# Attention scores from re-paired operand copies, double buffered, with the copies made by VectorE for ten heads and by DMA for 22

## The reference

```
scores = q @ k.T / 8 + min(cum[j] - cum[i], 0), cum = cumsum(max(s, 0)); -1e9 above the diagonal
attn   = softmax(scores);  out = attn @ v
```

## Time and profile before

| what | value |
|---|---|
| median of 3 runs | 968.08 us (964.08 to 968.49) |
| the profiled execution | 964.65 us, its span 962.9 us |
| TensorE busy | 911.1 us, 95% of the span |
| VectorE, ScalarE busy | 487.5 us (51%), 351.8 us (37%) |
| DMA | 159.34 MB, 165 GB/s |
| mean granted TensorE clock | 0.985 of 2.4 GHz |

### The profile page before, as it was taken

How to read it: one execution, slowest core, us unless ns; L and a number is a source line. 1 busy time by engine, 2 the same in 40 slices (tenths; PEclk the granted TensorE clock), 3 DMA queues, 4 the chain that set the end, 5 groups by cost and what they waited for, 6 DMA issues and landing times.

```text
span 962.9 us, 16180 instructions
## 1 busy us (share of the span) xinstructions
PE 911.1 (95%) x6455; PEld 856.4 (89%) x6455; DVE 487.5 (51%) x889; ACT 351.8 (37%) x670; POOL 37.7 (4%) x80
## 2 busy tenths in 40 slices
PE   1999899998999999999999999999999999999998
PEld 1777688977999999988999999989899999999998
DVE  5546779345554882445433784055534690342222
ACT  1445566344333642444232443243422341221111
POOL 2011000000000000001000000000000000000000
PEclk9979999997999999999999999999999999999999
DMA  4667565752664563745545445544655444444441
GB/s 96 155 186 228 158 162 179 235 181 66 218 226 160 175 207 116 250 131 159 191 150 176 150 131 169 175 131 119 206 187 176 173 150 159 175 149 164 176 175 50
DMA packets 70562, 159.34 MB, mean 165 GB/s; under 512 B 31892, under 2 KB 46228, under 8 KB 58200
## 3 DMA queue, kind: packets, MB, share of 16 engines
q1 hardware_dynamic: 68184, 154.66, 51.0%
q0 software_dynamic: 2304, 3.65, 1.3%
HBM read 118.11 MB, written 30.09 MB: 154 GB/s over the span
## 4 chain that ended last, share of the span: by engine, by line
PE 80%; DVE 10%; issue 3%; ACT 3%; SPq 1%; DMA 1%; ACTq 0%; DVEq 0%
PE psum L1101 21%; PE psum L1103 20%; PE psum L1102 20%; PE psum L1078 8%; PE psum L1024 3%; PE psum L1057 2%; PE psum L1055 2%; DVE neg_max L799 2%; PE psum L1038 1%; DVE work L865 1%; PE psum L1029 1%; PE psum L1062 1%; DVE sums L825 1%; DMA klc<-cum_scratch 1%; DVE work L868 1%
## 5 line engine op out<-in xcount | busy, mean ns | idle before, releaser
L1101 PE MATMUL psum<-uu_hl,ring 128*128 128x288 f32 x512 | 156.7, 306 | 6.3 <-DVE r_hl L908 2.1
L1101 PE MATMUL psum<-r_hl,ring 128*128 128x288 f32 x512 | 155.2, 303 | 2.1 <-ACT hid L666 1.1
L1103 PE MATMUL psum<-uu_hl,ring 128*128 128x288 f32 x512 | 152.0, 297 | 0.0
L1102 PE MATMUL psum<-uu_hl,ring 128*128 128x288 f32 x512 | 151.8, 296 | 0.0
L1103 PE MATMUL psum<-r_hl,ring 128*128 128x288 f32 x512 | 151.2, 295 | 0.0
L1102 PE MATMUL psum<-r_hl,ring 128*128 128x288 f32 x512 | 151.1, 295 | 0.0
L799 DVE TENSOR_REDUCE neg_max<-psum 128x1 f32<-128x512 f32 (+4 forms) x165 | 83.5, 539 | 106.7 <-PE psum L1029 100.7
L1078 PE MATMUL psum<-probs,va 128*128 128x320 f32 (+4 forms) x448 | 125.1, 390 | 2.7 <-ACT probs L629 2.7
L908 DVE SCALAR_TENSOR_TENSOR r_hl<-psum,r_hl 128x288 fp32r<-128x288 f32 x128 | 58.5, 457 | 125.0 <-ACT r_hl L712 124.5
L712 ACT ACTIVATE r_hl<-psum 128x288 fp32r<-128x288 f32 x128 | 52.5, 411 | 183.3 <-PE psum L1103 183.2
L1101 PEld LDWEIGHTS psum<-uu_hl,ring 128*128 128x128 f32 x512 | 97.4, 190 | 9.8 <-DVE uu_hl L903 3.7
(11 more groups left out here) (102 smaller groups left out, 1684.6 us busy)
## 6 DMA issues: line engine op xcount, KB each, us to landing
ring<-w_scratch SPq DMA_DIRECT2D x72, 1024.0 KB, 4.9
w_scratch<-ring SPq DMA_DIRECT2D x24, 1024.0 KB, 5.5
kq_raw<-in_kq_t SPq DMA_DIRECT2D x70, 288.0 KB, 4.2
stage<-in_w_ch SPq DMA_DIRECT2D x16, 512.0 KB, 4.9
khc<-khh SPq DMA_DIRECT2D x34, 144.0 KB, 2.3
qm<-qhl SPq DMA_DIRECT2D x34, 144.0 KB, 2.5
out_t<-u_acc SPq DMA_DIRECT2D x16, 288.0 KB, 5.8
va<-in_v SPq DMA_DIRECT2D x34, 128.0 KB, 3.8
```

Of the source, the lines that this page charges most:

```text
L1101: pe.matmul(o, hi, m_hi, start=start, stop=False)
L1102: pe.matmul(o, hi, m_lo, start=False, stop=False)
L1103: return pe.matmul(o, lo, m_hi, start=False, stop=stop)
```

## The change

- `khc`, `klc`, `khh`, `qhl`, `qm` become `kb`, `qb` (128 partitions) and `kc`, `qc` (97 partitions), all double. Now `kb` is k's low part above its high part, `qb` q's high part above its low part; `kc` and `qc` hold the high parts, two rows of cum, and in partition 96 the row of the maximum, rows between being constant. The scores are kb x qb + kc x qc; `max_scores` uses 66 rows of `kc` and `qc`, so cum has to be loaded into one place only. `kq_raw` is double.
- The high parts reach `kc` and `qc` by two VectorE copies (`highs`) for heads 0 to 9, in step 3, and for heads 10 to 31 by two DMAs (`load_highs`) issued in step 4 behind `load_v`; `max_scores` waits for them in the next step 0.
- The low parts are computed in step 3 (before: 2); `load` is issued in step 0 (before: 3), cum in step 2 alone.
- The maxima are not split: they are rounded to fp32r as they are written, and each transpose has a stationary operand of one column and gives one row.
- TensorE's order: scores 0, round 0, scores 1, round 1 in g = 0; values 0, scores 2, round 2 in g = 1; the transposes in g = 3, ahead of values 2. `keep_warm` is gone.
- The small loads (taps, U, V) move from before head 1 to step 4 of head 0, their splitting from (0, 3) to (2, 4). At the start both heads' k and q are loaded first.
- Nothing is done for heads past the last.

```diff
-        KROWS = D + 4
-        kq_raw = sb("kq_raw", [P, 2, S], F32)
-        k_raw, q_raw = kq_raw[:, 0, :], kq_raw[:, 1, :]
-        khh = [sb(f"khh{i}", [P, S], F32R) for i in range(2)]
-        qhl = [sb(f"qhl{i}", [P, S], F32R) for i in range(2)]
-        klc = [sb(f"klc{i}", [KROWS, S], F32R) for i in range(2)]
-        qm = [sb(f"qm{i}", [KROWS, S], F32R) for i in range(2)]
-        khc = sb("khc", [KROWS, S], F32R)
+        CROWS, KROWS = D + 2, 3 * P // 4 + 1
+        kq_raw = sb("kq_raw", [P, 2, 2, S], F32)
+        kb = [sb(f"kb{i}", [P, S], F32R) for i in range(2)]
+        qb = [sb(f"qb{i}", [P, S], F32R) for i in range(2)]
+        kc = [sb(f"kc{i}", [KROWS, S], F32R) for i in range(2)]
+        qc = [sb(f"qc{i}", [KROWS, S], F32R) for i in range(2)]
         va = [sb(f"va{i}", [P, NT, P], F32) for i in range(2)]
         probs = sb("probs", [P, 2, BANK], F32)
-        neg_max = sb("neg_max", [P, 8], F32)
-        max_split = sb("max_split", [P, NT, P], F32R)
+        neg_max = sb("neg_max", [P, 8], F32R)
+        WEIGHTS_HEADS = [1, 2, 4, 6]
+        SMALL_AT = (0, 4)
+        COPIED = H + 2
+        UV_AT = (2, 4)
                 def load(a, h):
-                    n = a * H + h
-                    ql_done.wait(sp, n - 1)
-                    kl_done.wait(sp, n - 1)
+                    n, i = a * H + h, h % 2
+                    if n >= B * H:
+                        return
+                    if n >= 2:
+                        ql_done.wait(sp, n - 2)
+                        kl_done.wait(sp, n - 2)
                     for half in (0, D):
-                        sp.dma_start(kq_raw[half:half + D, :, :], kq_t[source(a, h)]).then_inc(raw_in.sem, 16)
+                        sp.dma_start(kq_raw[half:half + D, i, :, :], kq_t[source(a, h)]).then_inc(raw_in[i].sem, 16)
                 def load_v(a, h):
                     n, i, c0 = a * H + h, h % 2, D * (h % 2)
+                    if n >= B * H:
+                        return
                     mm_pv.wait(sp, n - 2)
                     of = v[source(a, h)]
                     sp.dma_start(va[i][:, 0:NT - 1, c0:c0 + D],
                                  of[0:(NT - 1) * P, :].rearrange("(t p) d -> p t d", p=P)).then_inc(v_in[i].sem, 16)
                     sp.dma_start(va[i][P - D:P, NT - 1, c0:c0 + D], of[(NT - 1) * P:S, :]).then_inc(v_in[i].sem, 16)
-                def side(a, h):
+                def load_cum(a, h):
+                    n = a * H + h
+                    if n >= B * H:
+                        return
+                    mm_s.wait(sp, n - 2)
+                    sa, sh = source(a, h)
+                    sp.dma_start(kc[h % 2][D:D + 2, :].bitcast(F32), cum_scratch[sa * H + sh]).then_inc(cum_in.sem, 16)
+                def load_highs(a, h):
                     n, i = a * H + h, h % 2
+                    if n >= B * H:
+                        return
                     prep_hi.wait(sp, n)
-                    mm_max.wait(sp, n - 1)
-                    mm_s.wait(sp, n - 2)
-                    sp.dma_start(khc[0:D, :].bitcast(F32), khh[i][0:D, :].bitcast(F32)).then_inc(side_in.sem, 16)
-                    sp.dma_start(qm[i][0:D, :].bitcast(F32), qhl[i][0:D, :].bitcast(F32)).then_inc(side_in.sem, 16)
-                    sa, sh = source(a, h)
-                    cum = cum_scratch[sa * H + sh]
-                    sp.dma_start(khc[D + 2:D + 4, :].bitcast(F32), cum).then_inc(side_in.sem, 16)
-                    sp.dma_start(klc[i][D + 2:D + 4, :].bitcast(F32), cum).then_inc(side_in.sem, 16)
+                    sp.dma_start(kc[i][0:D, :].bitcast(F32), kb[i][D:2 * D, :].bitcast(F32)).then_inc(high_in.sem, 16)
+                    sp.dma_start(qc[i][0:D, :].bitcast(F32), qb[i][0:D, :].bitcast(F32)).then_inc(high_in.sem, 16)
+                def load_small():
...
                 def attention_step(a, h, g):
+                    if g == 0:
+                        load(a, h + 3)
                     if g == 2:
-                        side(a, h + 2)
-                    if g == 3:
-                        load(a, h + 3)
+                        load_cum(a, h + 2)
                     if g == 4:
                         load_v(a, h + 2)
+                        if a * H + h + 2 >= COPIED:
+                            load_highs(a, h + 2)
...
+                load(0, 0)
+                load(0, 1)
                 load_v(0, 0)
-                prep_hi.wait(sp, 0)
-                sp.dma_start(khc[0:D, :].bitcast(F32), khh[0][0:D, :].bitcast(F32)).then_inc(first_side, 16)
-                sp.dma_start(qm[0][0:D, :].bitcast(F32), qhl[0][0:D, :].bitcast(F32)).then_inc(first_side, 16)
-                load(0, 1)
-                for x, done in enumerate((s_cumh, s_cuml)):
-                    sp.wait_ge(done, 1)
-                    if x == 0:
-                        sp.wait_ge(s_rows, 3)
-                    row = y_hl[0][0:1, x, :].bitcast(F32)
-                    sp.dma_start(khc[D + 2 + x:D + 3 + x, :].bitcast(F32), row).then_inc(first_side, 16)
-                    sp.dma_start(klc[0][D + 2 + x:D + 3 + x, :].bitcast(F32), row).then_inc(first_side, 16)
+                for h in range(2):
+                    sp.wait_ge(s_rows1 if h else s_rows, 3)
+                    for x, done in enumerate((s_cumh, s_cuml)):
+                        sp.wait_ge(done, 1)
+                        sp.dma_start(kc[h][D + x:D + x + 1, :].bitcast(F32), y_hl[0][h:h + 1, x, :].bitcast(F32))\
+                          .then_inc(first_cum[h], 16)
...
+                    if (h, g) == SMALL_AT:
+                        load_small()
...
-                    raw_in.wait(act, n)
+                    if n >= B * H:
+                        return
+                    raw_in[i].wait(act, n // 2)
                     mm_s.wait(act, n - 2)
-                    act.activation(khh[i][:, :], k_raw, ACT.Copy).then_inc(prep_hi.sem, 1)
-                    act.activation(qhl[i][:, :], q_raw, ACT.Copy, scale=SCALE).then_inc(prep_hi.sem, 1)
+                    act.activation(kb[i][:, :], kq_raw[:, i, 0, :], ACT.Copy).then_inc(prep_hi.sem, 1)
+                    act.activation(qb[i][:, :], kq_raw[:, i, 1, :], ACT.Copy, scale=SCALE).then_inc(prep_hi.sem, 1)
                 def max_to_row(a, h):
                     n = a * H + h
+                    if n >= B * H:
+                        return
                     mm_mt.wait(act, n)
-                    act.activation(qm[h % 2][D:D + 2, :], psf[D:D + 2, MX:MX + S], ACT.Copy).then_inc(mrow.sem, 1)
+                    act.activation(qc[h % 2][KROWS - 1:KROWS, :], psf[0:1, MX:MX + S], ACT.Copy).then_inc(mrow.sem, 1)
...
+                    if g == 3:
+                        max_to_row(a, h + 1)
+                        prepare(a, h + 2)
                     if g == 4:
-                        max_to_row(a, h + 1)
...
-                def query_low(a, h):
+                def highs(a, h):
                     n, i = a * H + h, h % 2
+                    prep_hi.wait(dve, n, 1)
+                    dve.tensor_copy(kc[i][0:D, :], kb[i][0:D, :].bitcast(F32)).then_inc(copied.sem, 1)
                     prep_hi.wait(dve, n)
-                    dve.scalar_tensor_tensor(out=qhl[i][D:2 * D, :], in0=q_raw[D:2 * D], scalar=SCALE,
-                                             in1=qhl[i][D:2 * D, :].bitcast(F32), op0=ALU.mult, op1=ALU.subtract)\
+                    dve.tensor_copy(qc[i][0:D, :], qb[i][0:D, :].bitcast(F32)).then_inc(copied.sem, 1)
+                def lows(a, h):
+                    n, i = a * H + h, h % 2
+                    if n >= B * H:
+                        return
+                    if n < COPIED:
+                        copied.wait(dve, n, 1)
+                    else:
+                        prep_hi.wait(dve, n)
+                    dve.tensor_tensor(kb[i][0:D, :], kq_raw[0:D, i, 0, :], kb[i][0:D, :].bitcast(F32), ALU.subtract)\
+                       .then_inc(kl_done.sem, 1)
+                    dve.scalar_tensor_tensor(out=qb[i][D:2 * D, :], in0=kq_raw[D:2 * D, i, 1, :], scalar=SCALE,
+                                             in1=qb[i][D:2 * D, :].bitcast(F32), op0=ALU.mult, op1=ALU.subtract)\
                        .then_inc(ql_done.sem, 1)
-                def key_low(a, h):
-                    n = a * H + h
-                    mm_s.wait(dve, n - 2)
-                    dve.tensor_tensor(klc[h % 2][0:D, :], k_raw[0:D], khh[h % 2][0:D, :].bitcast(F32), ALU.subtract)\
-                       .then_inc(kl_done.sem, 1)
                 def maxima(a, h, r):
...
-                    if r == len(ROUNDS) - 1:
-                        red.wait(dve, n)
-                        dve.tensor_copy(max_split[:, :, D], neg_max[:, 0:NT]).then_inc(ms_hi.sem, 1)
-                        ms_hi.wait(dve, n)
-                        dve.tensor_tensor(max_split[:, :, D + 1], neg_max[:, 0:NT], max_split[:, :, D].bitcast(F32),
-                                          ALU.subtract).then_inc(ms_lo.sem, 1)
```

(62 more changed lines are left out.)

90 lines of the change are left out of this document (46 added, 44 removed).

## The result

The changed kernel takes 998.41 us (median of 4 runs, 996.64 to 999.54) against 966.92 us for the kernel before (4 runs, 964.08 to 968.49, on the same chip): a ratio of 1.034, 95% interval 1.032 to 1.037. It is slower, by more than the 990 forecast and within the range. The profiled execution took 997.98 us, span 995.8.

What follows compares the result with a forecast made beforehand. TensorE was taken as the bound from batch 1 on, a ring through three engines in batch 0. 964.65 - 5.2 + 2.6 - 8.1 + 27 + 8.4 = 989.4, given as 990 us; range 952 to 1011, forecast's own 975 to 1003.

Steps and rivals of the forecast that it cites:

- Start, -5.2: Up to the first scores: cum row issued and landing 4.7 us earlier, two splits gone; range -6 to -3.
- Batch 0, +2.6: Batch 0: 85.6 us against 83.0, paced by a ring through three engines; range -12 to +8.
- 2.0 over all: Batch 0: cum rows issued late, behind the 12 small loads or a stored block, cost 2.0 us in total.
- One stretch of 10.2: Batch 0: one stretch of 10.2 us at 0.50 clock, costing 5.1 us as before.
- ring: Batch 0: chain of dependent steps through three engines, 8.3 us per head, 66.4 us for eight heads.
- a head below 8: Batch 0: sign against the forecast, which is wrong if a head takes less than 8 us.
- Saved in batches 1 to 3, -8.1: Batches 1 to 3: round 2 and maximum-row waits go, transposes get shorter, maxima past the last head go; -8.1 us.
- The 2.9 for the maxima: Batches 1 to 3: three waits for line 799 go because round 2 moves a step later; 2.9 us saved.
- High parts by DMA, +27: Heads 10 to 31: step-4 DMAs behind `load_v` make TensorE wait; 31.1 us less 4 taken back, bounds 12 and 36.
- 14 for blocks: Seven of 22 DMA heads have a 0.5 to 1 MB load or store just ahead: 2 us each, 14.
- Clock, +8.4: Batches 1 to 3: three stretches of 10.2 us at half clock (15.3) instead of one costing 6.9; bounds -7 and +30.
- the clock goes with each wait: Rival, batches 1 to 3: new waits bring 1.2 GHz after nearly each, +30 us, 1011 us in all; chance 0.12.

Runs made afterwards that it cites:

- the fastest kernel: The changed kernel with batch 0's SyncE list rearranged, high-part DMAs in step 3, and heads 23 and 31 copied by VectorE: 954.16 us, ratio 0.9885.
- the other order of the list: The changed kernel with batch 0's small loads and weight blocks issued in step 2 behind the cum rows, instead of step 4: 983.24 us, ratio 1.017.
- the early DMAs: The changed kernel with the high-part DMAs issued in step 3 instead of step 4 behind the loads of v: 969.26 us, ratio 1.003.
- The two experiments: Keep-warm products put into the changed kernel with rearranged list and step-3 DMAs: 957.88 us, ratio 0.992; taken out of the kernel before: 975.12 us, ratio 1.009.

## Why the prediction was right, and where it was off

It was right in direction and in its largest term, and the total is 8 us short.

- **Start, -5.2.** Measured -6.3, just outside the range of -6 to -3. First product at 9.80, 6.2 before that of the earlier trace rows, so earlier than the near 11 I gave.
- **Batch 0, +2.6: the mis-sized step.** Measured +9.2, outside its range of -12 to +8. "2.0 over all" for late cum rows was 10.9, two waits of 5.4 and 5.6. I had seen both their causes (behind the small loads, behind a stored block) and priced the row at a quick landing. "One stretch of 10.2", 5.1, is in fact four (three are shown above), some 34 us at half clock, 27.0 of them busy; by half of the busy time (see the clock, below) some 13 is lost, an estimate. Set against the fastest kernel, which has 6.8 us at half clock in this batch and is busy 65.1, TensorE's 74.3 are 9.2 more. With the other order of the list cum cost 1.4 and the clock came to 0.89: both go together. The rest of my sum was too large and hid part of the miss: ring and additions without cum and low clock were 78.5, but the fastest kernel ran the whole batch in 75.1, with 1.3 of cum and some low clock in it. The second head, free of all additions on VectorE, took 8.1 beside the ring's 8.3, and the fifth, with two of a normalisation's, 7.8. I had said that a head below 8 would make the forecast wrong: one was, by 0.2, and it made no difference, so that test was drawn too tight.
- **Saved in batches 1 to 3, -8.1.** The rest of the kernel after the last head's start is 1.6 shorter (1.8 had been taken for the head past the last). Five transposes are 0.2 shorter (0.54 against 0.75 in the heads shown) where I took 0.1; over 23 heads that makes near 5 in place of 2.3. The 2.9 for the maxima had a wrong reason: round 2 stands one step behind round 1 in both kernels, so the order doesn't take that wait away. In the changed kernel it is near nothing (0.2), while round 0 waits for its DMAs; with the early DMAs 3.1 of it are back. Idle time of TensorE rose by 22.4 though the new waits are 29.8, so 7.4 of other waits went in all, where I had taken off 2.9, 1.1 and 4.
- **High parts by DMA, +27.** The waits are 29.8; my gross sum was 31.1, of which 4 were to be taken back. They stand at the heads named, and 1.0 each at two more. The experiment with the early DMAs confirms the chain that the term was built of: the two loads of v, the issues, the landing (2.68 to the use in the head shown, 2.5 in the earlier trace rows). The split was less good than the sum: the ten heads waited 27.7 where I had 17.1, and the other twelve 2.1. Values 3 to round 0 took 54.1 over the ten, where 41 stood in the sum, so most of what I had put down as 14 for blocks seems to have fallen on the ten. At heads 2 and 4 of batch 1 a block's store is issued just before `load_v` (166.44, 224.03), and values 3 to round 0 took 7.6 and 9.0 instead of the 4.3 of the head shown. The 2.3 us that the prediction adds from the Trainium skill (DMA: Bandwidth & Descriptors, on the anatomy of one DMA) are from a fit that the section gives for DMAs issued by GpSimd. These are issued by SyncE, and their medians are 2.5 before and 3.0 after, so the measurement decides.
- **Clock, +8.4: close by luck.** TensorE's busy time in heads 8 to 31 rose by 9.3, with ten stretches (58 us in all) at half clock instead of two (17). I had three stretches of 10.2, 30.6, and took half of their length. Most are short, 3.4 or 6.8, and nine of the ten begin beside a new wait or within 2 us behind it (one of the nine, at 224, was there before too). So of the rival "the clock goes with each wait" the mechanism largely came, but not its price of 30. What a stretch costs can be read off products of one shape in one of them and just behind it (the clock goes from 0.50 to 1.00 at 152.4; start, duration):

```profile
151.27 0.44 PE L1122 MATMUL psum<-x_hl,ring 128*128 128x288 f32 x1
151.51 0.44 PE L1123 MATMUL psum<-x_hl,ring 128*128 128x288 f32 x1
...
152.57 0.29 PE L1122 MATMUL psum<-x_hl,ring 128*128 128x288 f32 x1
152.71 0.29 PE L1123 MATMUL psum<-x_hl,ring 128*128 128x288 f32 x1
```

From start to start it is 0.24 at half clock and 0.14 at full. So near half of the busy time in a stretch is lost, and none of its idle time. TensorE is busy 47.2 of the 58 us (before: 15.6 of 17), 31.6 more; half is some 14 to 16, an estimate. The shorter transposes hide near 5 of that in the 9.3. My 8.4 for the clock and my 2.3 for the transposes were both too small, by amounts that partly cancel.
- **Heads 8 to 31 in sum.** The last three terms make 27.3; the ghost head's -1.8 lies behind the last head, so 29.1 stands against the 31.6 measured.
- **Keep-warm.** I took their 10.7 us of busy time as free gain beside the ring. The two experiments agree with this for the new order alone; in the old one they are worth 0.9%.

What stays open: how the 4.5 us which heads 8 to 31 still lack with the early DMAs divide (2.6 are idle time, 1.9 busy time, with 38 us at half clock instead of 17); what brings the clock down, in a list without long waits above all; and how much of batch 0's spread from 75.1 to 79.5 is chance, since each profile is one execution.

## What to carry to other kernels

A transfer has to be issued its whole latency ahead of its use, counted from where it stands in its queue's list and not from when its data is ready; here moving two issues one step, with the same bytes, was worth 27 us of 31.6. A few rows that the main engine needs go ahead of the bulk in the list, for a 4.5 KB row behind two megabytes took 8 us and was little better from another queue. And before moving work to a "free" place on an engine, read what that engine waits for there: its list is in order, and everything behind it inherits the wait.

## What was not expected of the hardware

- 4.5 KB were usable 8.06 us after their issue behind 2.1 MB on SyncE's queue, and 7.1 us after an issue from ScalarE, with the same blocks under way.
- TensorE ran 51.2 us in one piece at half clock (1.2 GHz) while it was busy in 47.4 of them; with 128 small products more in batch 0 there was no such stretch (0.94 for the batch instead of 0.70, one profile each).
- Transposing from one stationary column instead of 128 took 234 ns in place of 275 on the mean, and the load of the stationary operand 82 ns in place of 192 (medians); five together took 0.54 in place of 0.75 us.
- Half clock costs by busy time and not by length: products of one shape started 0.24 us apart in it and 0.14 just behind it, and 10.7 of the 58 us at half clock in heads 8 to 31 were idle anyway.
